# Attention and two mixtures of experts: the product with V as 384 moving columns over high and low halves of V

## The reference, cut to what matters

```python
q_bits = (einsum('bhsd,dk->bhsk', q, proj) > 0)      # B=2, H=8, S=768, D=64, 6 bits
k_bits = (einsum('bhsd,dk->bhsk', k, proj) > 0)
mask   = q_bucket[:, :, :, None] == k_bucket[:, :, None, :]
scores = where(mask, q @ k.T / sqrt(D), -1e9)
scores = scores - max(scores, -1)
attn   = exp(scores); attn = attn / (sum(attn, -1) + 1e-9)
x      = attn @ v                                    # then two mixtures of experts on x:
x      = moe(x, top 2 of 8);  x = moe2(x, top 1 of 8)   # 1536 rows, 512 -> 1024 -> 512
```

## Time and profile before

| | |
|---|---|
| median of 3 runs | 1042.85 us (1042.69 to 1044.78) |
| span of the profiled execution | 1064.0 us |
| its attention, first row maximum to last `head_out` | 19.4 to 347.6 us |
| TensorE busy over the span | 947.3 us (89%) |
| VectorE, ScalarE, GpSimd busy | 584.6 (55%), 340.6 (32%), 410.6 us (39%) |

### The profile page before, as it was taken

How to read it: one execution, slowest core, us unless ns; L and a number is a source line. 1 busy time by engine, 2 the same in 40 slices (tenths; PEclk the granted TensorE clock), 3 DMA queues, 4 the chain that set the end, 5 groups by cost and what they waited for, 6 DMA issues and landing times. The chain is left out here.

```text
span 1064.0 us, 19163 instructions
## 1 busy us (share of the span) xinstructions
PE 947.3 (89%) x5502; PEld 799.2 (75%) x5503; DVE 584.6 (55%) x1123; ACT 340.6 (32%) x548; POOL 410.6 (39%) x251
## 2 busy tenths in 40 slices
PE   6999999999999836999999999999564799999980
PEld 4889989988988634888888888888443588888870
DVE  5777777777775462544554544554337344454442
ACT  3556656655655401222111111221012124343000
POOL 1000000000000658746243333363264869895104
PEclk9999999999999956999999999999866899999995
DMA  8531341341340635645243433353285557775107
GB/s 270 132 97 42 107 117 37 103 126 37 103 143 16 241 137 199 207 142 177 81 165 117 123 125 118 120 191 114 68 249 188 198 188 257 236 245 179 40 30 247
DMA packets 112989, 152.02 MB, mean 143 GB/s; under 512 B 57792, under 2 KB 59840, under 8 KB 112960
## 3 DMA queue, kind: packets, MB, share of 16 engines
q1 hardware_dynamic: 80096, 64.08, 19.4%
q10 hardware_dynamic: 26624, 67.12, 19.3%
q0 software_dynamic: 6240, 20.45, 5.9%
HBM read 104.43 MB, written 47.19 MB: 142 GB/s over the span
## 5 line engine op out<-in xcount | busy, mean ns | idle before, releaser
L452 POOL TENSOR_TENSOR wring<-stage,wring 128x1024 f32 (+1 forms) x128 | 302.5, 2403 | 235.4 <-ACT wring L592 235.3
L592 ACT ACTIVATE wring<-stage 128x1024 f32 (+1 forms) x128 | 135.4, 1061 | 423.5 <-POOL wring L452 179.1
L1157 PE MATMUL bank<-wring,xT_hl 128*128 x352 | 144.9, 412 | 9.3 <-DVE xT_hl L890 9.3
L1037 PE MATMUL bank<-raw,work 128*128 128x64 f32 x1152 | 143.6, 275 | 3.2 <-ACT work L543 3.2
L1037 PEld LDWEIGHTS bank<-raw,work 128*128 128x128 f32 x1152 | 135.9, 191 | 12.9 <-issue 11.0
L1174 PE MATMUL bank<-wring,hT_hl 128*128 x352 | 141.6, 402 | 3.2 <-DVE hT_hl L909 3.2
L1159 PE MATMUL bank<-wring,xT_hl 128*128 x352 | 140.2, 398 | 0.0
L1158 PE MATMUL bank<-wring,xT_hl 128*128 x352 | 139.7, 397 | 0.0
L1176 PE MATMUL bank<-wring,hT_hl 128*128 x352 | 137.8, 391 | 0.0
L1175 PE MATMUL bank<-wring,hT_hl 128*128 x352 | 137.1, 390 | 0.0
L442 POOL TENSOR_TENSOR wring<-wring,ones 64x384 fp32r<-64x384 f32 x32 | 26.2, 820 | 287.2 <-ACT wring L528 287.2
(11 more groups left out here) (158 smaller groups left out, 1296.6 us busy)
## 6 DMA issues: line engine op xcount, KB each, us to landing
stage<-in_moe_w_dram ACTq DMA_DIRECT2D x128, 512.0 KB, 3.9
ys<-work SPq DMA_DIRECT2D x44, 256.0 KB, 3.1
work<-xs SPq DMA_DIRECT2D x40, 256.0 KB, 2.8
xs<-stage SPq DMA_DIRECT2D x7, 1024.0 KB, 4.5
raw<-in_k_dram SPq DMA_DIRECT2D x32, 192.0 KB, 3.3
raw<-in_q_dram SPq DMA_DIRECT2D x32, 192.0 KB, 3.6
ys<-stage SPq DMA_DIRECT2D x2, 1792.0 KB, 12.3
xs<-stage SPq DMA_DIRECT2D x7, 512.0 KB, 5.2
```

What stands on the lines that cost most here:

```text
L452: nc.gpsimd.tensor_tensor(wring[:, bass.ds(at + DC * F, GW)], stage[:, j % STAGES, :], wring[:, bass.ds(at, GW)].bitcast(F32), ALU.subtrac ...
L592: nc.scalar.activation(wring[:, bass.ds(parity * SLOT + high_at(j), GW)], stage[:, j % STAGES, :], ACT.Copy).then_inc(w_high, 1)
L1037: ins = mm(o_ps[:, j * D:(j + 1) * D], probsT[j % 2][:, i * P:(i + 1) * P], vraw[:, hp, i], start=i == 0, stop=i == QT - 1)
L1157: mm(o, xT_hl[:, 0, c, :], wh, start=c == 0, stop=False)
```

## The change

1. **The product with V.** The probabilities after the turn are no longer the stationary operand. They are split into a high part (`pT_high`, ScalarE, both halves of every tile) and the rest (`pT_low`, VectorE, both halves of every tile, which subtracts the high part from the PSUM value). V is split by GpSimd into 64 high and 64 low columns (`split_v`), which stand side by side as one stationary operand of 128 columns. `weigh` then moves three tiles (384 columns) through it at once, for the high part and for the rest, and is spread over three steps, with four matmuls in each. The output is turned the other way; `o_copy` on ScalarE takes it out of PSUM at j = 0 and 3, `turn_back` on TensorE turns it by three transposes at j = 4 and 5, and `head_out` on VectorE adds the V-high and V-low halves and divides.
2. **q and k together.** q and k of a row lie side by side, so that three transposes turn both (two units instead of four). The split gives `qk_top` and `qk_rest`, the bits take three matmuls a half instead of four, and one VectorE instruction a half writes the bits of both. Seven transfers within SBUF, issued by SyncE (`put_split`, `put_bits`), lay the parts into `q_hl`, `q_hb`, `k_hh` and `k_lb`. `scores` of a new head waits for them (`qk_put`).
3. **Row statistics.** The maximum is taken negated, so that the bias is a plain product of two columns instead of an operation with two products.

```diff
+            def put(to, at, n, t, row):
+                sp.dma_start(to[at:at + n, :].bitcast(F32), t[row:row + n, :].bitcast(F32)).then_inc(qk_put, 16)
+            def put_split(h, par):
+                sp.wait_ge(prep_ev, h * U + 2)
+                put(q_hl[par], 0, D, qk_top, 0)
+                put(k_hh[par], 0, D, qk_top, D)
+                put(q_hl[par], D, D, qk_rest, 0)
+                put(k_hh[par], D, D, qk_top, D)
+                put(q_hb[par], 0, D, qk_top, 0)
+                put(k_lb[par], 0, D, qk_rest, D)
+            def put_bits(h, par):
+                sp.wait_ge(prep_ev, h * U + 4)
+                put(q_hb[par], D, 2 * BITS, k_lb[par], QB)
...
+            def next_head(h, par):
+                put_split(h + 1, 1 - par)
+                load_qk(h + 2)
+                put_bits(h + 1, 1 - par)
+                sp.wait_ge(v_rdy, h * 2 + 2)
+                load_v(h + 2, par)
...
-            def evac(n, par, half, done):
-                act.wait_ge(pt_mm, n * 2 + (half + 1))
-                nc.scalar.activation(probsT[par][:, cols(half)], pt_ps[:, half, 0:HALF], ACT.Copy).then_inc(done, 1)
-            def evacs(n, j):
-                evac(n, j % 2, 0, pt_a)
-                if j % 2:
-                    evac(n, j % 2, 1, pt_b)
+            def pT_high(n, hh, j):
+                for half in range(2):
+                    act.wait_ge(pt_mm, n * 2 + (half + 1))
+                    if half == 0 and not (isinstance(hh, int) and hh < 2):
+                        act.wait_ge(s_pv, hh - 1)
+                    nc.scalar.activation(pT_top[j // KH][:, half * KH:(half + 1) * KH, at:at + P],
+                                         pt_ps[:, half, 0:HALF].rearrange("p (c n) -> p c n", n=P),
+                                         ACT.Copy).then_inc(pt_top, 1)
...
                     expo(n, j % 2, j, hp)
-                    if j or not first(h):
-                        evacs(n - 1, (j - 1) % QT)
+                    if j in (0, 3) and not first(h):
+                        o_copy(h * 2 - (2 if j == 0 else 1), 0 if j == 0 else 1)
+                    if j:
+                        pT_high(n - 1, h * 2 + (j - 1) // KH, j - 1)
...
+            def pT_low(n, j):
+                for half in range(2):
+                    dve.wait_ge(pt_top, n * 2 + (half + 1))
+                    vec.tensor_tensor(pT_rest[j // KH][:, c, at:at + P],
+                                      pt_ps[:, half, 0:HALF].rearrange("p (c n) -> p c n", n=P),
+                                      pT_top[j // KH][:, c, at:at + P].bitcast(F32), ALU.subtract).then_inc(pt_rdy, 1)
...
                     stats(n, j % 2)
-                    if j == 1 and not first(h):
-                        head_out(h - 1, 1 - hp)
-                    if j % 2:
-                        evac(n - 1, 0)
+                    if j >= U and not first(h):
+                        head_out(h - 1, 1 - hp, j - U)
+                    if j:
+                        pT_low(n - 1, j - 1)
...
-            def weigh(n, j, h, hp):
-                    ins = mm(o_ps[:, j * D:(j + 1) * D], probsT[j % 2][:, i * P:(i + 1) * P], vraw[:, hp, i],
-                             start=i == 0, stop=i == QT - 1)
+            def weigh(hh, b, h, hp, part):
+                for i in (2 * part, 2 * part + 1):
+                    mm(o_ps, v_hl[hp][:, i], pT_top[b][:, i], start=i == 0, stop=False)
+                    ins = mm(o_ps, v_hl[hp][:, i], pT_rest[b][:, i], start=False, stop=i == QT - 1)
+            def turn_back(hh, b, h):
+                for i in range(KH):
+                    ins = nc.tensor.transpose(misc_ps[:, i * P:(i + 1) * P], o_flat[b][:, i * P:(i + 1) * P], ident[:])
```

More of the change, by code:

```diff
@@ L283, in last @@
             return isinstance(h, int) and h == H - 1
[L286 to L288 removed]
+        U = 4
+        PUTS = 7
+        S_O0 = 2
         def prep_bank(h, u):
[L292 removed]
+            return banks[3][:, 0, :] if first(h) and u % 2 else misc_ps
         def cols(half):
@@ L435, in _, with split_v, head @@
             nc.gpsimd.iota(tri_in[:], [[1, E], [-1, E]], base=0, channel_multiplier=0, **io).then_inc(pool_c, 1)
[L437 to L446, removed]
+            def split_v(h, par, part):
+                c = slice(part % 2 * KH, (part % 2 + 1) * KH)
+                vr = vraw[:, par, c]
+                if part < 2:
+                    if part == 0:
+                        pool.wait_ge(v_ld[par], (h // 2) * 16 + 16)
+                        if not (isinstance(h, int) and h < 2):
+                            pool.wait_ge(s_pv, h * 2 - 2)
+                    one = ones[:, 0:KH * D].rearrange("p (c d) -> p c d", d=D) if KH * D <= P else \
+                        ones[:, 0:1].unsqueeze(1).broadcast_to([P, KH, D])
+                    nc.gpsimd.tensor_tensor(v_hl[par][:, c, 0:D], vr, one, ALU.mult).then_inc(v_top, 1)
+                else:
+                    pool.wait_ge(v_top, h * 2 + (part - 1))
+                    nc.gpsimd.tensor_tensor(v_hl[par][:, c, D:2 * D], vr, v_hl[par][:, c, 0:D].bitcast(F32),
+                                            ALU.subtract).then_inc(v_rdy, 1)
+            def head(h, hp):
+                for j in range(4):
+                    split_v(h, hp, j)
+            over_heads(pool, head)
             def low_part(g, parity, pieces=range(GRAN)):
@@ L730, in head @@
                         inverse_sums(h - 1, 1 - hp)
-                    if not last(h):
+                    if not last(h) and j < U:
                         prep_unit(h + 1, 1 - hp, j)
-                    if j == 1 and not first(h):
-                        head_out(h - 1, 1 - hp)
-                    if j % 2:
-                        evac(n - 1, 0)
+                    if j >= U and not first(h):
+                        head_out(h - 1, 1 - hp, j - U)
+                    if j:
+                        pT_low(n - 1, j - 1)
+                    elif not first(h):
+                        pT_low(n - 1, QT - 1)
             over_heads(dve, head)
             inverse_sums(H - 1, (H - 1) % 2)
-            head_out(H - 1, (H - 1) % 2)
+            pT_low(H * QT - 1, QT - 1)
+            for half in range(2):
+                head_out(H - 1, (H - 1) % 2, half)
             def bc(ap, shape, *axes):
@@ L978, in prep_unit @@
             def prep_unit(h, par, u):
-                what, half = PREP[u]
+                half = u % 2
                 if not first(h):
-                    pe.wait_ge(prep_ev, h * U + u)
+                    if u:
+                        pe.wait_ge(prep_ev, h * U + u)
+                    elif not (isinstance(h, int) and h < 2):
+                        pe.wait_ge(s_o, h * 2 - (4 - S_O0))
                 elif u >= 2:
@@ L1063, in _ @@
             over_heads(pe, head)
-            nn = H * QT
-            turn(nn - 1, 1)
-            weigh(nn - 2, QT - 2, H - 1, 1)
-            weigh(nn - 1, QT - 1, H - 1, 1)
+            weigh(2 * H - 2, 0, H - 1, 1, 2)
+            turn(H * QT - 1, 1)
+            for part in range(3):
+                weigh(2 * H - 1, 1, H - 1, 1, part)
+            for b in range(2):
+                turn_back(2 * H - 2 + b, b, H - 1)
             def route(m):
                 ne = 2 * E if m == 0 else E
-                pe.wait_ge(s_o, H)
+                pe.wait_ge(s_o, S_O0 + H * 2)
                 for t in range(TT):
```

229 lines of the change are left out of this document (122 added, 107 removed).

## The result

The changed kernel takes **1114.9 us** (median of 4 runs, 1113.29 to 1116.99) against 1043.82 of the kernel before: a ratio of **1.0685** (95% interval 1.0663 to 1.0706), 71 us slower. The forecast was 1134 us, with a range of 1095 to 1175. The span of its profile is 1111.4 us.

What follows compares the result with a forecast made beforehand. TensorE bound the kernel at 20.44 us a head; a closed round of 4.10 us a step would make it 25.7. Fifteen heads +79, last head +10, start +2 gave +91 on 1042.85: 1134 us, range 1095 to 1175.

Steps and rivals of the forecast that it cites:

- the closed round: Attention step: stats, expo, pT_high, pT_low, next stats wait for each other in order; 4.10 us a step; held 78%.
- The step of 4.10 us: One attention step: 1.45 to the exponential, 0.99 for it, 0.54 for pT_high's first half, 1.12 for subtractions; bounds 3.79 to 4.24.
- the two subtractions: VectorE's pT_low, two a step until the next row maximum: 2 times 0.56, 1.12 us.
- The handover within the 0.54: From pT_high's first half on ScalarE to VectorE: copy 0.43 us plus handover 0.11.
- The 0.2 for GpSimd: split_v on GpSimd holding up VectorE instructions: 0.2 us a head, 0 to 0.8.
- Start and last head: Start: first scores wait for seven transfers, +2 us (0 to +5); last head: work in a row, +10 (+8 to +12).
- VectorE by load alone: Rival: the round doesn't close and VectorE's load binds at 19.3 us a head, 1033 us, faster; 6%.
- The clock did fall: Rival: pauses in every step bring TensorE's clock down in the attention, +137, 1180 us; 8%.
- The 0.32 us between score matmuls: Spacing near the start instead of 0.18, used to price TensorE at the lower clock: 28.6 us a head instead of 16.0.
- TensorE's share: Sign in the profile after: TensorE about 60 to 65% busy in the attention.
- Late transfers: Rival: put_bits needs 11.6 us instead of under 9.8, each head waits 1.8 us, +27, 1161 us; 8%.
- a matmul of the bits: TensorE's preparation of q and k: 0.35 us each, six instead of eight a head, 2.1 us.

Runs made afterwards that it cites:

- The swapped order: The changed kernel with pT_high(n-1) ahead of expo(n) on ScalarE instead of behind it: 1036.7 us, 0.9938 of the kernel before.
- the two fillers: The changed kernel with 64 unread copies added, on VectorE between prep_unit and pT_low: 1111.4 us; in another run on ScalarE between expo and pT_high: 1137.4 us.
- the run with the clock held up: The changed kernel with four more unread float32 matmuls of 128 columns on TensorE ahead of each group of three tiles: 1107.0 us.
- the kernel with 64 rows: The changed kernel with the second of the three matmuls of the bits over 64 rows instead of 128: 1119.8 us.

## Why the prediction was right

**The bound before, and the order after.** Both held. TensorE set the pace before; after, the closed round of `stats`, `expo`, `pT_high`, `pT_low` does. The swapped order and the two fillers show it, against VectorE's load and ScalarE's load, and the run with the clock held up shows it against the clock.

**The step of 4.10 us** was mis-sized by 0.22. Of its terms 1.45, 0.99 and 0.54 came out as 1.45, 0.98 and 0.51; the two subtractions, put at 1.12, need 0.94 until the next maximum starts, because the first leaves 0.47 us for the second to start, although it lasts 0.55. That overlap stood in the rows (L708, 0.46) and I took it for the lower bound only. The handover within the 0.54 was sized wrong too, with no effect: a copy lasts 0.49 and the subtraction starts 0.02 later, where I had 0.43 and 0.11. Fifteen heads at 6 × 0.22 are 20 us, and by size that is the whole distance from 1134 to 1114.9; the terms below nearly cancel.

**The rest of a head.** `o_copy` was put at 0.43 and is 0.38. The 0.2 for GpSimd came out as a number by luck: 24.25 is 0.2 above 6 × 3.88 + 2 × 0.38, but only because head 0, without `o_copy` and with a first step of 1.93, takes 21.59. The fourteen heads of the loop take 24.44, 0.4 above. Of this 0.4, two thirds stand at j = 1 and 4, with the clock down. The other third, 0.13 a head, stands at j = 3 and is GpSimd's: while it splits V, the last instruction of `stats` (L744) takes up to 0.54 us instead of 0.16, and the exponential behind it starts that much later, in a step of 4.64:

```profile
177.42 0.95 DVE L738 TENSOR_REDUCE stat<-bank 128x1 f32<-128x768 f32 x1
177.59 0.97 POOL L482 TENSOR_TENSOR wring<-raw,ones 128x192 fp32r<-128x192 f32 x2 [22.59 <-PE bank L1088]
178.52 1.14 POOL L485 TENSOR_TENSOR wring<-raw,wring 128x192 fp32r<-128x192 f32 x2
178.59 0.54 DVE L744 TENSOR_TENSOR stat<-stat 128x1 f32<-128x1 f32 x1
```

With the clock held up these steps went back to 4.26 as well, where GpSimd starts 0.2 us before the step and L744 takes 0.16 to 0.18 us in all heads but one (0.24). In the last head it is seen again: the product of `head_out` (L771, 1.49 us in the rows above) takes 0.36 alone, and ran beside GpSimd's first work on the weights (L498, from 415.64 us). Both instructions have two SBUF inputs, so this agrees with the exclusive port pair of the Trainium skill, "SBUF — State Buffer", sections Terms and Who interferes with whom; the subtractions, with one input in PSUM, took 0.55 or 0.56 us each throughout.

**Start and last head.** +2.3 and +11.2 against +2 and +10. The second is near by offsetting errors: the five rounds took 20.5 us instead of 21.4 (which holds two copies of 0.43, as it should, and not the one that its sentence names), and what follows them 12.3 instead of 10.4, of which 1.1 is that product.

**The rivals.** VectorE by load alone was put at 19.3 us a head; with the order swapped it is 19.25. As a forecast of the change as made it was rightly the small chance; as a price of the next bound it hit the number, in part by luck: VectorE's busy time is 17.6 us a head there and not 19.1, since instructions in a row overlap by nearly 0.1 us, and the rest of 19.25 is gaps inside `stats` and single waits. The clock did fall, to 0.86 to 0.91, which I had named as a sign against the forecast; but it cost at most 8 us, not 137, since TensorE has slack in the round. The rule of the Trainium skill on short pauses ("TensorE: Matmul & The Clock Gate", section A second HAM failure mode: psum-queue depth-cycling) described this going up and down rightly; the trace adds its small price here. The 0.32 us between score matmuls was the right price, though the earlier trace rows are a weak source for it: the granted clock at 20 us reads 1.00. In the changed kernel matmuls of 384 columns start 0.32 us apart at a granted clock of 0.50 (219.16 and 219.48 us). The other sign that missed is TensorE's share: 60 to 65% was forecast and 77% measured (230.4 of 300 us), part of it matmuls slowed by the clock. Late transfers stayed hidden while a head took 24 us, and came out at 18 to 19 us a head, as a queue behind clears: at the first heads in the swapped order, in the loop as well with the edit of q and k alone.

**One price was wrong and didn't matter.** I counted a matmul of the bits at 0.35 us, from the earlier trace rows; it takes 0.18 once all of them use 128 rows. TensorE wasn't the bound. For the edit of q and k alone this matters: eight at 0.35 before against six at 0.175 after are 1.75 us a head.

Not settled: why the clock stayed down longer in the kernel with 64 rows, and what makes the part behind the attention take 716 to 721 us in some executions and 693 in others, with the same code there.

## What to carry to other kernels

When a piece of work moves to engines that have room, don't ask for their load first but write down, for one step, who waits for whom in written order, and follow it until it closes; the sum along that circle is the step, however idle the engines are. If an instruction stands behind another that it doesn't need, exchange the two before giving up the change: here that alone was worth 78 us. And when a stage gets faster, look again at the transfers it had hidden, and at what is queued ahead of them.

## What the runs showed of the hardware

- At the upper clock, float32r matmuls of 384 columns over 128 and 64 rows in turn start 0.27 to 0.35 us apart, all over 128 rows 0.17 to 0.18; 128 and 76 rows in turn (the scores) also keep 0.17 to 0.18.
- With two pauses of about 1.7 us in a head of 24 us, the granted clock of the attention was 0.86 to 0.91; with four small matmuls in each it was 1.00. In the swapped order, where the pauses are 0.7 us at most, it was 1.00 too.
- A one-column VectorE operation with two SBUF inputs took up to 0.54 us instead of 0.16 beside GpSimd's work, and one of 192 columns 1.49 instead of 0.36; a subtraction of 384 columns with one input in PSUM kept 0.55.
- VectorE starts a second instruction of 0.55 us 0.47 us after the first when nothing between them waits.
- Six transfers of 192 KB within SBUF are issued in 3.8 us, in 5.8 to 6.6 behind a clear, and in 8.4 at 25 us, behind two of 1792 KB.
